# A tiled squared-ReLU attention ahead of two feed-forward layers: order of the products in an attention step, a tile's last step in two parts, another start

## The chip, the cores and the metric

The program runs on one core of a Trainium2 chip. The metric is the device time of one execution in microseconds (us), less is better. The engines are TensorE (PE; its weight loads are PEld), VectorE (DVE), ScalarE (ACT), GpSimd (POOL) and SyncE (SP), which issues nearly all the DMAs. Each works through its own instructions in order, and they wait for each other by semaphores.

## What is computed

```python
def _attn_ref(u, v, z):                     # u, v: (2, 3008, 256)   z: (2, 3008, 64)
    scores = (1.0 / 3008) * np.matmul(z, z.transpose(0, 2, 1))
    attn = np.maximum(scores, 0.0) ** 2
    return u * np.matmul(attn, v)

def _moe_ref(x, w_in, w_out):               # x: (6016, 256), 2048 hidden
    h = x @ w_in
    return (h - np.tanh(h)) @ w_out

def _moe2_ref(x, w_gate, w_val, w_out):     # 1536 hidden
    gate = 1.0 / (1.0 + np.exp(-(x @ w_gate)))
    return (gate * (x @ w_val)) @ w_out

def reference(...):
    return _moe2_ref(_moe_ref(_attn_ref(u, v, z).reshape(6016, 256), ...), ...)
```

## The kernel before

Every matmul operand is split in two: a high half (a rounded copy in fp32r) and a low half (what the rounding left). A product is three matmuls: high by high, high by low, low by high.

**Attention.** Twelve tiles `T` of 512 queries (448 in tiles 5 and 11), six per batch, each over 12 steps `p` of two chunks of 128 keys; `s = 12 T + p` counts 144 steps. `score(s)` (L428) computes z by z into two banks of `hidden`: a contraction of 64, so the matmuls come in pairs, one on the upper 64 rows of the array and one on the lower, three pairs a step. `attend(s)` (L453) multiplies the squared scores by v into `acc`: twelve pairs a step, three for each key chunk `c` and each half `d` of the output's 256 columns. The rows of a chunk are shared between the two array halves, so each `d` has two partial sums, `acc[d]` and `acc[2 + d]`. In a tile's last step 64 keys are padding and nine pairs do. PE's order is written by hand: `score(s + 2)`, then `attend(s)` (L584).

Between them ACT takes the relu of the scores (L712, "relu" below, into `first`, profile name `h`), waits until `attend(s - 2)` is done, and squares it into `part_hi` (L724, "square"). DVE squares in full precision (L902, into `full`, profile name `h`) and subtracts the high half from it, into `part_lo` (L915, by the helper at L799; "low half" below). `attend(s)` waits for the low half (`s_alo`, L476) before its first pair, since its second pair needs it.

**A tile's border.** When tile T is done, its partial sums are joined: ACT copies `acc[2 + d]` into `x_out` (L636), DVE adds `acc[d]` (L851, `s_sum`), d = 0 then 1. ACT does its copies in step 13 of the tile's count (`GATE_AT`: the next tile's p = 1) between relu and square, DVE its sums at the start of that step. The first half is signalled by PE (`s_half`) after five of the last step's nine pairs. PE may write the next tile's `acc[d]` only after `s_sum` (L479). One step later DVE multiplies by u (`gate_by_u`, L860), and SP stores the tile and loads the next u (L387).

**Beside it,** z and v are staged by DMA through three buffers and split into halves by "tasks" (ACT L624, DVE L799; table at L121): a task comes first in its step. The scores of tile 0 wait for the low half of z (L439). The weights of both layers are combined and split in the free time of DVE and ACT (`weight_steps`, L146; DVE L811 to L817 and L799) and stored by SP as `ready`; each unit's raw weights are loaded three steps ahead (L392).

**The start.** GpSimd clears `part_lo` (L613), and PE runs 8 warm-up pairs of 512 columns on it (L578), which compute nothing that is used, then `score(0)`, which waits for ACT's high half and later for DVE's low half of the first z piece.

**The two layers** follow (L589 on): products of x by weights into `hidden` (`product`, L424 to L426), activations on ACT and DVE, and second products into `acc`. The change leaves them alone.

## Time and profile before

| | us |
|---|---|
| three runs | 1509.5, 1510.15, 1510.15; median 1510.15 |
| the profiled execution | 1509.4 |
| its span, first to last instruction | 1507.6 |

| engine | busy, us | share of the span |
|---|---|---|
| PE | 1496.5 | 99% |
| PEld | 1312.2 | 87% |
| DVE | 1138.6 | 76% |
| ACT | 948.7 | 63% |

A pair of matmuls is recorded at some 0.39 us, but the next pair starts 0.23 us after it: matmuls are pipelined. So a gap in PE's work that is shorter than 0.16 us shows in no idle time, and a longer one shows shortened. It is seen from the starts of neighbouring rows, and from the idle time of PEld. The attention takes the first 486 us.

### The profile page before, as it was taken

Reading aid. Unit: us, or ns where it says so; the run is one execution under the profiler, and the core shown is the slowest. Engines: PE = TensorE matmul, PEld = TensorE weight load, DVE = VectorE, ACT = ScalarE, POOL = GpSimd, SP = SyncE. Lnnn points to the kernel's source line nnn. Section 1 sums busy time; section 2 is a strip of 40 time slices with the busy share of each in tenths; the row PEclk is TensorE's granted clock in tenths of the full one; section 3 lists DMA queues with packets and bytes.
Section 4 is the critical chain, followed back from the end, with each engine's and each line's share of the span. In section 5 each row is a group of like instructions: output and inputs, shape, how many; then the busy total and the mean of one; then the engine's idle time right before and its main releaser. Section 6 shows DMA issues by size and latency. Waiting matters only on the chain.

```text
span 1507.6 us, 21886 instructions
## 1 busy us (share of the span) xinstructions
PE 1496.5 (99%) x8800; PEld 1312.2 (87%) x8800; DVE 1138.6 (76%) x1409; ACT 948.7 (63%) x1282; POOL 0.7 (0%) x5
## 2 busy tenths in 40 slices
PE   9999999999999999999999999999999999999998
PEld 7999999999999788888888889888888888888897
DVE  8898888999987777767776767666666676666655
ACT  7676667767666666666666666656555555555654
POOL 0000000000000000000000000000000000000000
PEclk9999999999999999999999999999999999999999
DMA  4334432245333345354535446543635454554352
GB/s 133 130 124 154 154 120 88 104 168 219 126 120 142 122 149 209 125 200 154 188 137 191 157 158 233 201 174 140 241 129 208 162 195 175 189 184 183 135 207 87
DMA packets 36325, 241.79 MB, mean 160 GB/s; under 512 B 3584, under 2 KB 6656, under 8 KB 22912
## 3 DMA queue, kind: packets, MB, share of 16 engines
q1 hardware_dynamic: 36080, 240.17, 43.5%
q8 instruction: 69, 1.13, 0.3%
q14 instruction: 32, 0.26, 0.1%
q10 hardware_dynamic: 144, 0.23, 0.0%
HBM read 196.21 MB, written 44.17 MB: 159 GB/s over the span
## 4 chain that ended last, share of the span: by engine, by line
PE 98%; DVE 1%; ACT 0%; issue 0%; POOLq 0%; DVEq 0%
PE acc L470 25%; PE hidden L424 12%; PE hidden L426 12%; PE hidden L425 12%; PE acc L424 10%; PE acc L425 10%; PE acc L426 10%; PE hidden L447 6%; DVE part_lo L799 0%; PE acc L578 0%; DVE h L868 0%; DVE h L902 0%; ACT snap L665 0%; DVE region L799 0%; DVE h L894 0%
## 5 line engine op out<-in xcount | busy, mean ns | idle before, releaser
L799 DVE TENSOR_TENSOR part_lo<-h,part_hi 128x1024 fp32r<-128x1024 f32 (+2 forms) x315 | 375.4, 1192 | 91.8 <-ACT part_hi L676 49.4
L470 PE MATMUL acc<-part_hi,region 64*128 64x512 f32 (+1 forms) x2256 | 398.2, 384 | 2.0 <-DVE part_lo L799 1.6
L665 ACT ACTIVATE snap<-hidden 128x512 f32<-128x512 f32 (+1 forms) x360 | 211.7, 588 | 253.8 <-PE hidden L426 253.7
L424 PE MATMUL hidden<-region 128*128 128x512 f32 (+1 forms) x840 | 324.4, 386 | 2.6 <-ACT snap L665 1.9
L426 PE MATMUL hidden<-region 128*128 128x512 f32 (+1 forms) x840 | 323.7, 385 | 0.0
L425 PE MATMUL hidden<-region 128*128 128x512 f32 (+1 forms) x840 | 323.7, 385 | 0.0
L868 DVE TENSOR_TENSOR h<-hidden,snap 128x512 f32<-128x512 f32 (+1 forms) x252 | 170.9, 678 | 148.7 <-ACT snap L665 122.3
L470 PEld LDWEIGHTS acc<-part_hi,region 64*128 64x128 f32 x2256 | 258.5, 184 | 14.4 <-issue 7.0
L424 PE MATMUL acc<-part_hi,region 128*128 128x512 f32 (+1 forms) x672 | 259.2, 386 | 0.2 <-DVE part_lo L799 0.2
L425 PE MATMUL acc<-part_lo,region 128*128 128x512 f32 (+1 forms) x672 | 259.0, 385 | 0.0
L426 PE MATMUL acc<-part_hi,region 128*128 128x512 f32 (+1 forms) x672 | 258.9, 385 | 0.0
L470 PE MATMUL acc<-part_lo,region 64*128 64x512 f32 (+1 forms) x1128 | 250.5, 382 | 0.0
L724 ACT ACTIVATE part_hi<-h 128x1024 fp32r<-128x1024 f32 (+1 forms) x143 | 149.2, 1044 | 136.3 <-PE acc L470 136.1
L676 ACT ACTIVATE part_hi<-h 128x1024 fp32r<-128x1024 f32 (+1 forms) x166 | 172.9, 1042 | 81.5 <-DVE h L972 42.5
L424 PEld LDWEIGHTS hidden<-region 128*128 128x128 f32 x840 | 157.7, 188 | 35.0 <-ACT snap L665 3.7
L426 PEld LDWEIGHTS hidden<-region 128*128 128x128 f32 x840 | 157.7, 188 | 29.6
L425 PEld LDWEIGHTS hidden<-region 128*128 128x128 f32 x840 | 157.7, 188 | 29.4
L902 DVE TENSOR_TENSOR h<-h 128x1024 f32<-128x1024 f32 (+1 forms) x143 | 171.0, 1196 | 0.2 <-ACT h L712 0.2
L424 PEld LDWEIGHTS acc<-part_hi,region 128*128 128x128 f32 x672 | 126.1, 188 | 24.5 <-DVE part_lo L799 0.5
L426 PEld LDWEIGHTS acc<-part_hi,region 128*128 128x128 f32 x672 | 126.2, 188 | 23.8
L425 PEld LDWEIGHTS acc<-part_lo,region 128*128 128x128 f32 x672 | 126.2, 188 | 23.7
L712 ACT ACTIVATE h<-hidden 128x1024 f32<-128x1024 f32 (+1 forms) x143 | 141.6, 990 | 0.5 <-PE hidden L447 0.5
(56 smaller groups left out, 1185.7 us busy)
## 6 DMA issues: line engine op xcount, KB each, us to landing
region<-ready SPq DMA_DIRECT2D x33, 2304.0 KB, 8.8
region<-ready SPq DMA_DIRECT2D x51, 1408.0 KB, 6.0
ready<-region SPq DMA_DIRECT2D x6, 2304.0 KB, 7.4
ready<-region SPq DMA_DIRECT2D x8, 1408.0 KB, 5.6
xs<-x_out SPq DMA_DIRECT2D x20, 512.0 KB, 4.9
x_in<-xs SPq DMA_DIRECT2D x20, 512.0 KB, 7.9
snap<-vP SPq DMA_DIRECT2D x24, 256.0 KB, 2.7
u_in<-uT SPq DMA_DIRECT2D x10, 512.0 KB, 5.1
```

Of the source, the lines that this page charges most:

```text
L424: pe.matmul(dst, w_hi, x_hi, start=start, stop=False, skip_group_check=True)
L425: pe.matmul(dst, w_hi, x_lo, start=False, stop=False, skip_group_check=True)
L426: return pe.matmul(dst, w_lo, x_hi, start=False, stop=stop, skip_group_check=True)
L447: last = pe.matmul(hidden[:, 2 * (s % 2) + c, 0:w], keys_of[ROWS[c], keys], tokens_of[ROWS[c], tokens], start=i == 0, stop=i == 2, skip_gr ...
L470: last = pe.matmul(acc[:, 2 * r + d, 0:w], v[ROWS[r], 2 * p + c, half], a[ROWS[r], 2 * (s % 2) + c, 0:w], start=start, stop=False, skip_gr ...
L665: act.activation(snap[:, g % 2, i, 0:w], hidden[:, CHAIN[g % 2], 0:w], ACT.Copy).then_inc(s_snap, 1)
L676: act.activation(part_hi[:, b, 0:w], h[:, n % 2, b, 0:w], ACT.Copy).then_inc(s_hi, 1)
L712: act.activation(first[:, k, :, 0:w], hidden[:, 2 * k:2 * k + 2, 0:w], ACT.Relu, scale=1.0 / SEQ).then_inc(s_relu, 1)
L724: act.activation(part_hi[:, 2 * k:2 * k + 2, 0:w], first[:, k, :, 0:w], ACT.Square).then_inc(s_ahi, 1)
L799: return ve.tensor_tensor(dst, whole, hi.bitcast(F32), ALU.subtract)
L868: ve.tensor_tensor(dst, hidden[:, (BANK2, BANK7, BANK7)[i], 0:w], snap[:, g % 2, (0, 2, 1)[i], 0:w], ALU.add).then_inc(s_add, 1)
L902: ve.tensor_tensor(full[:, k, :, 0:w], first[:, k, :, 0:w], first[:, k, :, 0:w], ALU.mult).then_inc(s_full, 1)
```

## The change

The products of an attention step are put in another order: all that need the high half of the squared scores first (`highs`, two pairs each), then those that need the low half (`lows`, one pair). `highs` waits for `s_ahi` (ACT's square), `lows` for `s_alo`. Tile-first steps go by d, so that each d waits for its own `s_sum`.

A tile's last step is cut in two, after its fifth pair, where `s_half` is signalled, and `score(s + 2)` stands between the parts. ACT's copy of the first half moves ahead of the relu of the GATE_AT step; DVE's first sum moves one step earlier, between the full square and the low half of the next tile's first step; the second copy and sum stay in the GATE_AT step. `gate_by_u`, `store_tile` and `load_u` come one step later. The weights' and the second batch's tasks get other steps (`EARLY`, `late`, `X0_SPLIT`), none of them in the two steps around a border.

At the start the first z piece is split by DVE alone (a copy, then the subtraction, signalled by `s_zhi`), and the warm-up is 12 pairs of 256 columns on a half-size clear.

```diff
 NSTAGE = 3
-WARM = 8
+WARM = 12
...
+def steps_between(a, b):
+    return [s for s in range(a, b) if s not in GATE_AT and s + 1 not in GATE_AT]
+EARLY = steps_between(14, 60)
 def split_tasks():
...
     tasks += [(p, "v", (0, p)) for p in range(1, STEPS)]
-    tasks += [(at, "z", (1, k)) for k, at in enumerate((19, 31, 43, 55, 63, 65))]
-    later = [at for at in range(67, 81) if at not in GATE_AT and at - 1 not in GATE_AT]
-    tasks += [(at, "v", (1, p)) for p, at in enumerate(later)]
+    tasks += [(EARLY[5 * k + 4], "z", (1, k)) for k in range(ZP)]
+    tasks += [(at, "v", (1, p)) for p, at in enumerate(steps_between(67, 81))]
     return sorted(tasks, key=lambda t: t[0])
...
 def weight_steps():
-    free = [s for s in range(81, 125) if s not in GATE_AT and s - 1 not in GATE_AT]
+    late = steps_between(81, X0_LOAD)
     for k, pieces in enumerate(WPIECES):
         if WLAYER[k] == 0:
-            yield tuple(15 + 6 * k + i for i in range(2 + pieces))
+            yield tuple(EARLY[5 * k:5 * k + 4])
         else:
-            yield tuple(free.pop(0) for _ in range(2 + pieces))
+            yield tuple(late.pop(0) for _ in range(2 + pieces))
+X0_LOAD, X0_SUMS = 125, 127
+X0_SPLIT = (131, 134, 135, 136, 137, 138, 139)
 WSTEPS = tuple(weight_steps())
 WEIGHTS_AT = {s: (k, i) for k, steps in enumerate(WSTEPS) for i, s in enumerate(steps)}
-X0_LOAD, X0_SUMS = 125, 127
-X0_SPLIT = (131, 132, 135, 136, 137, 138, 139)
 assert max(WEIGHTS_AT) < X0_LOAD
...
                 for T in range(NT - 1):
-                    if s == GATE_AT[T] + 2:
+                    if s == GATE_AT[T] + 3:
                         store_tile(T)
...
                     piece = -(-2 * P * (p + 1) // ZW) - 1
-                    if p == 0 and T == 0:
-                        pe.wait_ge(s_thi, TASK_NUMBER["z", (b, piece)] + 1)
+                    if s == 0:
+                        pe.wait_ge(s_zhi, 1)
                     else:
...
-            def attend(s):
+            def pair(s, upper, lower, start=False):
...
                 w = tile_width(T)
...
+            def wait_v(s):
+                T, p = ORDER[s]
                 if T == 0 or T == TPB:
...
-                for c, d in whole:
-                    pe.wait_ge(s_alo, c + 1 if s == 0 else behind(s))
-                    if p == 0 and c == 0 and T > 0:
+            def highs(s, c, d):
+                T, p = ORDER[s]
+                pe.wait_ge(s_ahi, c + 1 if s == 0 else behind(s))
+                pair(s, (d, c, vh, part_hi), (d, c, vh, part_hi), p == 0 and c == 0)
+                return pair(s, (d, c, vl, part_hi), (d, c, vl, part_hi))
+            def lows(s, c, d):
+                pe.wait_ge(s_alo, c + 1 if s == 0 else behind(s))
+                return pair(s, (d, c, vh, part_lo), (d, c, vh, part_lo))
+            def attend(s):
+                T, p = ORDER[s]
+                wait_v(s)
+                if s == 0:
+                    for c in range(2):
+                        for d in range(DH):
+                            highs(s, c, d)
+                        for d in range(DH):
+                            last = lows(s, c, d)
+                elif p == 0:
+                    for d in range(DH):
                         pe.wait_ge(s_sum, 2 * (T - 1) + d + 1)
-                    if p == STEPS - 1 and c == 1:
-                        pair((0, c, vh, part_hi), (0, c, vh, part_lo))
-                        pair((0, c, vl, part_hi), (1, c, vl, part_hi)).then_inc(s_half, 1)
-                        continue
-                    for v, a in ((vh, part_hi), (vh, part_lo), (vl, part_hi)):
-                        last = pair((d, c, v, a), (d, c, v, a), p == 0 and c == 0 and v is vh
-                                    and a is part_hi)
-                if p == STEPS - 1:
-                    last = pair((1, 1, vh, part_hi), (1, 1, vh, part_lo))
+                        for c in range(2):
+                            highs(s, c, d)
+                        for c in range(2):
+                            last = lows(s, c, d)
+                else:
+                    for c in range(2):
+                        for d in range(DH):
+                            highs(s, c, d)
+                    for c in range(2):
+                        for d in range(DH):
+                            last = lows(s, c, d)
                 last.then_inc(s_attn, 1)
+            def attend_end_first(s):
+                wait_v(s)
+                highs(s, 0, 0)
+                lows(s, 0, 0)
+                pair(s, (0, 1, vh, part_hi), (0, 1, vh, part_lo))
+                pair(s, (0, 1, vl, part_hi), (1, 1, vl, part_hi)).then_inc(s_half, 1)
+            def attend_end_second(s):
+                highs(s, 0, 1)
+                lows(s, 0, 1)
+                pair(s, (1, 1, vh, part_hi), (1, 1, vh, part_lo)).then_inc(s_attn, 1)
             def product(n, s, i):
...
                 for r in range(2):
-                    pe.matmul(acc[:, 2 * r, :], part_lo[ROWS[r], 0, 0:P], part_lo[ROWS[r], 0, :],
-                              start=True, stop=True, skip_group_check=True)
+                    pe.matmul(acc[:, 2 * r, 0:256], part_lo[ROWS[r], 0, 0:P],
+                              part_lo[ROWS[r], 0, 0:256], start=True, stop=True,
+                              skip_group_check=True)
             score(0)
...
             for s in range(1, NSTEP - LAG):
-                score(s + LAG)
-                attend(s)
+                if ORDER[s][1] < STEPS - 1:
+                    score(s + LAG)
+                    attend(s)
+                else:
+                    attend_end_first(s)
+                    score(s + LAG)
+                    attend_end_second(s)
             attend(NSTEP - 2)
-            attend(NSTEP - 1)
+            attend_end_first(NSTEP - 1)
+            attend_end_second(NSTEP - 1)
             products_begin(0, 0)
...
-            gp.memset(part_lo[:, 0, :].bitcast(F32), 0.0).then_inc(s_zero, 1)
+            gp.memset(part_lo[:, 0, 0:256].bitcast(F32), 0.0).then_inc(s_zero, 1)
...
-            def copy_halves(T):
+            def copy_half(T, d):
...
                 for task in tasks_at(s):
-                    split_task(task)
+                    if task > 0:
+                        split_task(task)
+                if s in GATE_AT:
+                    copy_half(GATE_AT.index(s), 0)
                 if s == 0:
...
                 if s in GATE_AT:
-                    copy_halves(GATE_AT.index(s))
+                    copy_half(GATE_AT.index(s), 1)
                 act.wait_ge(s_relu, behind(s))
...
             def split_task(k):
                 whole, hi, lo = staged(k)
-                ve.wait_ge(s_thi, k + 1)
+                if k == 0:
+                    ve.wait_ge(s_stage[0], 16)
+                    ve.tensor_copy(hi, whole).then_inc(s_zhi, 1)
+                    ve.wait_ge(s_zhi, 1)
+                else:
+                    ve.wait_ge(s_thi, k)
                 minus(lo, whole, hi).then_inc(s_tlo, 1)
             def sum_weights(k, i):
...
-            def sum_halves(T):
+            def sum_half(T, d):
...
                 if s in GATE_AT:
-                    sum_halves(GATE_AT.index(s))
+                    sum_half(GATE_AT.index(s), 1)
                 if s == 0:
...
                     split_x(0, X0_SPLIT.index(s))
+                if s + 1 in GATE_AT:
+                    sum_half(GATE_AT.index(s + 1), 0)
                 ve.wait_ge(s_full, behind(s))
...
                       part_hi[:, 2 * k:2 * k + 2, 0:w]).then_inc(s_alo, 1)
-                if s - 1 in GATE_AT:
-                    gate_by_u(GATE_AT.index(s - 1))
+                if s - 2 in GATE_AT:
+                    gate_by_u(GATE_AT.index(s - 2))
```

In PE's order at the first border, from the score of step 13 (before) or from the last whole step of tile 0 (after), to the next tile's first step; `hidden` rows are scores, `acc` rows are `attend`. Before:

```order
L447 MATMUL hidden<-region 128x512 x6
L470 MATMUL acc<-part_hi,region 128x512 x2
L470 MATMUL acc<-part_lo,region 128x512 x2
L470 MATMUL acc<-part_hi,region 128x512 x3
L470 MATMUL acc<-part_lo,region 128x512
L470 MATMUL acc<-part_hi,region 128x512 x4
L470 MATMUL acc<-part_lo,region 128x512 x2
L470 MATMUL acc<-part_hi,region 128x512 x3
L470 MATMUL acc<-part_lo,region 128x512
L447 MATMUL hidden<-region 128x512 x6
L470 MATMUL acc<-part_hi,region 128x512 x2
```

After:

```order
L468 MATMUL acc<-part_hi,region 128x512 x4
L468 MATMUL acc<-part_lo,region 128x512 x2
L468 MATMUL acc<-part_hi,region 128x512
L468 MATMUL acc<-part_lo,region 128x512
L468 MATMUL acc<-part_hi,region 128x512 x2
L455 MATMUL hidden<-region 128x512 x6
L468 MATMUL acc<-part_hi,region 128x512 x4
L468 MATMUL acc<-part_lo,region 128x512 x2
L468 MATMUL acc<-part_hi,region 128x512
L468 MATMUL acc<-part_lo,region 128x512
L455 MATMUL hidden<-region 128x512 x6
L468 MATMUL acc<-part_hi,region 128x512 x8
```

The score of step 13 has moved from before the last step into its middle.

In DVE's order at the same border (the `x_out` rows are the sums and, at 128x2x512, the product by u; `h` is the full square, `raw` are weights). Before:

```order
L902 TENSOR_TENSOR h<-h 128x1024
L799 TENSOR_TENSOR part_lo<-h,part_hi 128x1024
L851 TENSOR_TENSOR x_out<-acc,x_out 128x512 x2
L902 TENSOR_TENSOR h<-h 128x1024
L799 TENSOR_TENSOR part_lo<-h,part_hi 128x1024
L902 TENSOR_TENSOR h<-h 128x1024
L799 TENSOR_TENSOR part_lo<-h,part_hi 128x1024
L860 TENSOR_TENSOR x_out<-x_out,u_in 128x2x512
```

After:

```order
L955 TENSOR_TENSOR h<-h 128x1024
L904 TENSOR_TENSOR x_out<-acc,x_out 128x512
L847 TENSOR_TENSOR part_lo<-h,part_hi 128x1024
L904 TENSOR_TENSOR x_out<-acc,x_out 128x512
L955 TENSOR_TENSOR h<-h 128x1024
L847 TENSOR_TENSOR part_lo<-h,part_hi 128x1024
L955 TENSOR_TENSOR h<-h 128x1024
L865 TENSOR_TENSOR raw<-raw 128x128
L866 TENSOR_TENSOR raw<-raw 128x128
L847 TENSOR_TENSOR part_lo<-h,part_hi 128x1024
```

The first sum now stands ahead of the low half of step 12, the second behind it.

DVE's first instructions, before and then after:

```order
L799 TENSOR_TENSOR region<-snap,region 128x512 x3
L894 TENSOR_TENSOR h<-h 128x512
L799 TENSOR_TENSOR part_lo<-h,part_hi 128x512
L894 TENSOR_TENSOR h<-h 128x512
L799 TENSOR_TENSOR part_lo<-h,part_hi 128x512
```

```order
L854 CAST region<-snap 128x512
L847 TENSOR_TENSOR region<-snap,region 128x512 x3
L947 TENSOR_TENSOR h<-h 128x512
L847 TENSOR_TENSOR part_lo<-h,part_hi 128x512
L947 TENSOR_TENSOR h<-h 128x512
```

One instruction is added ahead of the three subtractions.

## Rows read from the trace of the kernel before

**Rows 1.** The page: engines' totals; then one of PE's waits: us, times, longest.
```profile
PE 1496.5 (99%) x8800; PEld 1312.2 (87%) x8800; DVE 1138.6 (76%) x1409; ACT 948.7 (63%) x1282; POOL 0.7 (0%) x5
...
PE acc L470 <- DVE part_lo L799: 1.6, 1, 1.6
```

**Rows 2.** Idle time before attend's PE instructions, in us, and the number of times.
```profile
  issue: 7.0, 13
```

**Rows 3.** Timeline, first border: start us, duration us, engine, instruction [idle before].
```profile
47.59 0.88 PE L447 MATMUL hidden<-region 64*128 64x512 f32 x6
47.89 1.06 ACT L724 ACTIVATE part_hi<-h 128x1024 fp32r<-128x1024 f32 x1 [1.43 <-PE acc L470]
...
48.85 1.01 ACT L712 ACTIVATE h<-hidden 128x1024 f32<-128x1024 f32 x1
...
49.76 0.59 ACT L636 ACTIVATE x_out<-acc 128x512 f32<-128x512 f32 x1
...
50.31 0.88 PE L447 MATMUL hidden<-region 64*128 64x512 f32 x6
50.38 1.49 DVE L851 TENSOR_TENSOR x_out<-acc,x_out 128x512 f32<-128x512 f32 x2
...
51.22 0.50 PE L470 MATMUL acc<-part_hi,region 64*128 64x512 f32 x2
51.52 0.43 PE L470 MATMUL acc<-part_lo,region 64*128 64x512 f32 x2
```

**Rows 4.** Timeline of PEld where it restarts behind tiles 1 and 5.
```profile
91.63 0.21 PEld L470 LDWEIGHTS acc<-part_hi,region 64*128 64x128 f32 x2 [0.42 <-issue]
...
249.90 0.22 PEld L470 LDWEIGHTS acc<-part_hi,region 64*128 64x128 f32 x2 [0.50 <-issue]
```

**Rows 5.** Timeline of PE, two undisturbed steps apart.
```profile
54.04 0.87 PE L447 MATMUL hidden<-region 64*128 64x512 f32 x6
...
55.17 0.64 PE L470 MATMUL acc<-part_hi,region 64*128 64x512 f32 x4
55.63 0.42 PE L470 MATMUL acc<-part_lo,region 64*128 64x512 f32 x2
...
57.44 0.87 PE L447 MATMUL hidden<-region 64*128 64x512 f32 x6
```

**Rows 6.** Groups by line and shape, attention: count | busy us, mean ns.
```profile
L799 DVE TENSOR_TENSOR part_lo<-h,part_hi 128x1024 fp32r<-128x1024 f32 x119 | 145.8, 1225 | 32.4 <-ACT part_hi L724 30.3
...
L851 DVE TENSOR_TENSOR x_out<-acc,x_out 128x512 f32<-128x512 f32 x20 | 13.8, 692 | 2.5 <-ACT x_out L636 0.8
```

**Rows 7.** The chain that ended last, up to 16.4 us: start us, us, what.
```profile
1.31 3.78 PE acc L578 x12
...
6.19 0.60 ACT h L703
...
6.81 0.70 DVE h L894
...
15.67 0.61 DVE region L799
```

**Rows 8.** Timeline of the start.
```profile
3.55 1.28 ACT L624 ACTIVATE region<-snap 128x512 fp32r<-128x512 f32 x2 [1.53 <-DMA snap<-zT]
...
4.89 1.94 PE L447 MATMUL hidden<-region 64*128 64x512 f32 x12
...
5.87 0.69 DVE L799 TENSOR_TENSOR region<-snap,region 128x512 fp32r<-128x512 f32 x1 [0.31 <-ACT region L624]
```

**Rows 9.** Timeline of PEld at the start of the attention's last step.
```profile
484.41 0.19 PEld L470 LDWEIGHTS acc<-part_hi,region 64*128 64x128 f32 x2 [0.24 <-DVE part_lo L799]
...
484.72 0.39 PEld L470 LDWEIGHTS acc<-part_hi,region 64*128 64x128 f32 x3
```

**Rows 10.** SP's timeline: a load of raw weights behind a border.
```profile
379.21 0.86 SPq L316 DMA_DIRECT2D x_in<-w  x1
```

**Rows 11.** The page's DMA issues: count, KB each, median us to landing.
```profile
x_in<-w SPq DMA_DIRECT2D x3, 1280.0 KB, 8.3
```

55 lines of the change are left out of this document (25 added, 30 removed).

## The prediction

> **What bounds the kernel now.** Start with the totals: PE is busy for 1496.5 of 1507.6 us, DVE for 76% [rows 1]. So no edit that leaves PE's products alone can bring more than the few us in which PE stands still or runs slowly. The list of waits names almost nothing for the attention (1.6 us behind DVE at the start [rows 1]), but it hides short gaps, since a pair of matmuls is drawn at 0.39 us and the next starts earlier. So the pitch comes next: from one score to the next score an undisturbed step takes 57.44 - 54.04 = 3.40 us for 15 pairs, 0.2267 us a pair [rows 5]. Against that pitch the timeline of a tile's border is read [rows 3]. The score of step 14 starts at 50.31; three pairs later, at 50.99, `attend(12)` could start. It starts at 51.22, 0.23 late, and its second pair follows after 0.30 instead of 0.23 (an emptied PE needs 0.07 to refill). That is 0.30 us lost. What ended last: DVE's first sum, 50.38 plus 0.69 [rows 6] = 51.07, and 0.15 until PE moves. PE's weight loads restart from 0.42 us idle at the next border too, and from 0.50 behind tile 5 [rows 4]; attend's instructions have 13 such gaps with 7.0 us idle in all [rows 2], eleven at the eleven borders and two at the start. Lost at the borders: 10 x 0.30 + 0.38 = 3.4 us.
>
> The start is a second place. PE runs warm-up until the first score at 4.89 [rows 8], and from 6.81 to 16.29 the chain of waits runs through DVE alone: sums of squares, low halves, splits of z and v, with no PE in it [rows 7]. Then PE gets the next z piece at 16.4. Third: `attend(143)`, the last step, waits for its low half: PEld idles 0.24 us at 484.41, and the pair behind comes 0.31 later instead of 0.20, some 0.17 us lost in all [rows 9].
>
> **The change part by part.** *The border.* I lay the new order on the old times, from 47.59, where attend(10) ends [rows 3]. PE: five pairs of attend(11), of which the fifth (it signals `s_half`) starts at 48.50 and has drained at 48.92; three pairs of score, to 49.41; four pairs of attend(11), to 50.31; three of score, to 50.99; then attend(12). No pair is added. ACT: the square of step 12 runs 47.89 to 48.95 as before [rows 3], so the copy, now ahead of the relu, runs 48.96 to 49.55. DVE's first sum (0.69) ends at 50.27; with 0.15 to PE it is there at 50.42, and 50.99 is when it is wanted: 0.57 to spare, where 0.23 was missing. Then DVE must do the low half of step 12 (1.23 [rows 6]): 50.24 to 51.47, with 0.15 at PE at 51.62. In the old order of products that would have stopped PE again, since its second pair needs it at 51.22. In the new one, four pairs of high halves go first and it is wanted at 51.90: the two parts of the change need each other. ACT's second copy comes behind the relu (scores drained 49.60, relu to 50.65, copy to 51.2), DVE's second sum behind the low half: 51.4 to 52.1, at PE 52.25. The second d starts six pairs into the step, at 52.35. With the 0.07 of refill that is a tie: the cost lies between 0 and 0.07 us a border. I take 0.02, because each time above is rounded against the change. Border: 3.4 - 11 x 0.02 = **3.2 us** won; ends 2.6 and 3.4.
>
> *The moves around it.* ACT's copy now stands ahead of a relu that PE's later scores wait for; that relu comes 0.8 later than at 48.85 and is wanted only by score(15), at 53.7. Behind DVE's new wait (some 1.5 us idle for the copy) are queued the low half of step 12, the second sum and the full square of step 13. DVE leaves the border about 1.3 us behind its old times. It is wanted by PE for low halves, which are now needed eight pairs (1.8 us) into a step, and it has 3.40 us for 2.45 us of squares and low halves plus 0.6 to 0.9 of splitting; `gate_by_u` (1.2 us) moves one step back, still before the backlog reaches 1.8 + 1.4 us of slack. So 0. `store_tile`, `load_u` and, queued behind them on SP, the raw weights of the units that load there come about 3.4 us later. The tightest of them is the unit of 1280 KB whose load issues at 379.21 [rows 10]: it comes to stand directly behind the product by u and two DMA issues (1.3 us), a load of its size and place lands 8.3 us after its issue [rows 11], and its first use is three steps and a full square (10.2 + 1.2) after that product. So 9.6 us of 11.4 are used: the cover is 1.8 us, and if it is gone, DVE stands still, and PE only once the low half is 1.8 us later still. Cost 0, price if wrong: about 1 us for each of five such loads.
>
> *The order inside a step.* Same pairs, same weights, other banks: PE changes the `acc` bank after one or two pairs instead of three. Unknown as such; the nearest rows are four matmuls that cross a bank, 55.17 to 55.63, 0.46 for two pairs [rows 5], which is the 0.23 of any pair. Taken 0; bounds -0.2 and +0.5 us over all.
>
> *The start.* The copy that DVE adds is not in the trace. Its bounds are nothing and a subtraction of the same tile, 0.69 [rows 8]; I take the upper end. DVE starts when ACT did, at 3.55: high half 4.25, PE's first score pair at 4.4; low half 4.95, second pair 5.1, third 5.5 at the half-speed pitch of 0.43 that the warm-up shows (the relu now starts 1.29 after the first pair, two such pitches and one drain), relu at 5.95 instead of 6.19 [rows 7]. DVE is then busy with the third split until 6.56 [rows 8], so its first square starts at 6.57 instead of 6.81. From there on the chain is DVE's and 0.24 is carried through to 16.4; one relu that it met at its own end comes earlier too, for 0.1 more. That PE runs attend(0) and attend(1) about 1 us earlier (high halves come before low halves) brings nothing, because the next score waits for DVE's split of z. Start: **0.3 us** won; ends 0 and 0.9.
> The Trainium skill (VectorE: DVE Perf Modes, "The perf-mode tier table") has a 32-bit copy in SBUF at twice the rate of a `tensor_tensor`; by it the copy would be an estimated 0.4 us, the relu would start 0.1 earlier, ACT's third split would then hold it, and the start would be worth 0.3 still. No row here shows that copy.
>
> *The attention's last step.* The low half is wanted two pairs later, by more than it was late: **0.17 us** won.
>
> Sum: 3.2 + 0.3 + 0.2 = 3.7 us. 1509.4 of the profiled execution, 1.8 of it outside the span, becomes 1505.7. The four times of the kernel before have a mean of 1509.8, 0.35 under the median; I forecast **1506.1** for the median after. In the two layers nothing is changed, and PE's few gaps there are behind its own products, so they move with it.
>
> **The rivals.** *The second sum replaces the first.* If the tie above goes against the change by 0.1 to 0.2 us (a copy that waits longer behind the relu, a wait that costs DVE 0.1), each border keeps 0.15 us: gain 3.7 - 1.5 = 2.2, 1507.6. For it: the slack of 0.03. Against it: only that sum is so tight, and eleven borders are alike.
> *The clock.* Eight warm-up pairs take 3.78 us [rows 7], 0.43 each: 512 columns at 1.2 GHz. The six pairs of the first two scores take 1.94 [rows 8], which is two pitches of 0.43, three of 0.23 and a drain, so PE works at 2.4 GHz from about 5.7 us, after 4.4 us without a gap. The new warm-up ends near 3.9 us and leaves PE idle for 0.5 before the first score. If the rise comes later for that, each pair at the lower level costs 0.2 more, but up to 16 us PE has over 1 us in hand. A rise at 9 us costs under 0.2, one at 12.5 about 0.4: 1506.3 to 1506.5.
> The Trainium skill (TensorE: Matmul & The Clock Gate, "The HAM clock gate") says that the moment of the rise varies between runs; the one trace here can't show that.
> *The change does not do what it says:* PE's gap is at the border for another reason than the first sum, such as the order of banks or the square. Then the borders stay as they are: 1509.3. Against it: 51.07 and 51.22 are 0.15 apart, the distance of every start of PE behind DVE.
> *Slower.* PE pays for changing the `acc` bank. There are some four more changes a step, in 144 steps 570; from 6 ns each the gain of 3.7 is gone, and at 12 ns the time is 1509.8 + 3.1 = 1513. For it: no stretch of this kernel changes banks with every pair as the low halves now do. Against it: two pairs across a change take 0.46 [rows 5].
> *More.* The start goes by PE and not by DVE: 0.9 instead of 0.3, 1505.5; a small chance.
>
> **How the numbers follow.** About 0.2%, 3.0 us, is what a measurement of this kernel can tell from no change. Forecast (1505.3 to 1507.0): 0.57, all but 0.04 of it faster by over 0.2%. Second sum: 0.20, two thirds of it within 0.2%. Late clock: 0.06, half of it within. More: 0.06, faster. Not what it says, or a late DMA that eats the gain: 0.06, within. Slower: 0.05. Sum: faster 0.69, same 0.26, slower 0.05; one third of the cases are short of the forecast and few beyond it, so the range is lopsided: 1505.0 to 1508.7, which leaves out half of "more", the case without gain and the slower one.
>
> **What would show it.** In the profile after: PEld's idle time before attend's instructions at the borders gone (7.0 us down to under 3); the distance from tile to tile down from 91.63 - 51.19 (weights loaded 0.03 ahead of the 51.22 of [rows 3]) = 40.44 to 177 pairs x 0.2267 = 40.13 us; the first sum ended some 0.6 us before attend(12) starts; no gap six pairs into that step; PE's start behind the first z wait at 16.1 instead of 16.4; no gap at the attention's last step; the pitch of a step still 3.40. The forecast is wrong if the pitch is above 3.41, if a gap stands at each border's fourth or sixth pair, or if DVE's waits for raw weights show up.

## The result, and the profile after

| | before | after |
|---|---|---|
| median, us (20 runs each) | 1509.62 | 1507.05 |
| lowest and highest | 1508.47, 1510.15 | 1506.24, 1509.03 |
| the profiled execution, and its span | 1509.4, 1507.6 | 1506.3, 1504.5 |
| first product of the layers starts | 486.43 | 484.24 |

The ratio is 0.9985, 95% interval 0.9979 to 0.9991: 2.6 us faster, 0.17%. That is a gain that can be measured, but less than the 3.7 us forecast, and just under the 0.2% that the prediction counted as faster. The time lies 1 us above the number forecast and inside the range.

**The borders.** The first border again, now of the kernel after (start us, duration us, engine, instruction [idle before]):

```profile
47.51 1.06 ACT L771 ACTIVATE part_hi<-h 128x1024 fp32r<-128x1024 f32 x1 [1.43 <-PE acc L468]
...
48.36 0.87 PE L455 MATMUL hidden<-region 64*128 64x512 f32 x6
48.59 0.60 ACT L680 ACTIVATE x_out<-acc 128x512 f32<-128x512 f32 x1
...
49.22 0.69 DVE L904 TENSOR_TENSOR x_out<-acc,x_out 128x512 f32<-128x512 f32 x1 [1.58 <-ACT x_out L680]
...
49.82 1.22 DVE L847 TENSOR_TENSOR part_lo<-h,part_hi 128x1024 fp32r<-128x1024 f32 x1
49.95 0.87 PE L455 MATMUL hidden<-region 64*128 64x512 f32 x6
...
50.63 1.10 PE L468 MATMUL acc<-part_hi,region 64*128 64x512 f32 x8
...
50.96 0.69 DVE L904 TENSOR_TENSOR x_out<-acc,x_out 128x512 f32<-128x512 f32 x1
...
51.53 0.64 PE L468 MATMUL acc<-part_lo,region 64*128 64x512 f32 x4
...
51.99 0.87 PE L468 MATMUL acc<-part_hi,region 64*128 64x512 f32 x6
```

Against [rows 3]: the score starts at 49.95 and `attend(12)` at 50.63, three pairs of 0.227 later, with no gap. The first sum ended at 49.91, 0.72 early, where in [rows 3] PE had to wait 0.23 for it. The second sum ends at 51.65, and the second d starts at 51.99, six pairs after 50.63: it was a tie on paper and is none in the trace. The low half ends at 51.04 and is wanted at 51.53. So the four pairs of high halves, the two of low halves and the second d follow each other at an even pitch, and the changes of the `acc` bank cost nothing.

What attend's weight loads waited for, over the whole kernel after (us, times):

```profile
  DVE part_lo L847: 2.0, 1
  DVE region L847: 1.0, 1
```

The 7.0 us in 13 places of [rows 2] are gone. One new entry of 2.0 us stands there, and it is the surprise of this case.

**The new gap.** Timeline of SP, DVE and PE of the kernel after, at steps 124 to 128; then the same place of the kernel before:

```profile
418.06 0.55 SPq L372 DMA_DIRECT2D xs<-x_out  x1
418.65 0.62 SPq L376 DMA_DIRECT2D u_in<-uT  x1
419.86 0.33 SPq L330 DMA_DIRECT2D ready<-region  x1
420.31 2.11 SPq L367 DMA_DIRECT2D x_in<-xs  x2
...
433.08 0.69 DVE L885 TENSOR_TENSOR x_in<-x_in 128x512 f32<-128x512 f32 x1 [5.35 <-DMA x_in<-xs]
...
434.97 1.20 PE L468 MATMUL acc<-part_lo,region 64*128 64x512 f32 x8 [1.56 <-DVE part_lo L847]
```

```profile
418.39 0.55 SPq L364 DMA_DIRECT2D xs<-x_out  x1
418.99 0.62 SPq L368 DMA_DIRECT2D u_in<-uT  x1
423.14 0.33 SPq L322 DMA_DIRECT2D ready<-region  x1
423.59 1.31 SPq L359 DMA_DIRECT2D x_in<-xs  x2
...
433.56 0.69 DVE L831 TENSOR_TENSOR x_in<-x_in 128x512 f32<-128x512 f32 x1 [1.60 <-DMA x_in<-xs]
```

`load_x(0)` fetches the first batch's rows for the layers; DVE adds them up from step `X0_SUMS` = 127 on. Before, its first transfer was issued 4.6 us behind the u load, and the second landed 9.55 us after its own issue. After, `store_tile` and `load_u` stand one step later, directly ahead of it: it is issued 1.7 us behind the u load, with the tile's store (landed 421.41), the u load (423.80), a `ready` store and its own two halves all under way at once, and the second lands 12.27 us after its issue (420.79 to 433.06). Before, the u load had landed at 423.50, ahead of the first transfer's issue. DVE sits idle for 5.35 us in front of the first row sum. The low half of step 127 is queued behind that sum, ends at 434.9, and PE has stood still since its last high half: the starts of neighbouring pairs are 2.02 apart at 432.95, then 0.34. That is 1.9 us lost once per execution.

**The start.** Timeline of the kernel after:

```profile
3.53 0.43 DVE L854 CAST region<-snap 128x512 fp32r<-128x512 f32 x1 [3.53 <-DMA snap<-zT]
...
4.01 2.77 PE L455 MATMUL hidden<-region 64*128 64x512 f32 x12
...
16.13 0.96 PE L455 MATMUL hidden<-region 64*128 64x512 f32 x6 [1.62 <-DVE region L847]
```

The z wait ends at 16.13 instead of 16.42, the 0.3 us of the forecast. DVE's copy took 0.43 us.

**From the two traces to the medians.** To the start of the layers: 486.43 - 484.24 = 2.2 us. Read from the starts of all pairs, the borders gave 3.7, the start 0.3, the last step 0.2, and the new gap took 1.9: 2.3. The layers themselves, from their first product to the last (1502.82 before, 1499.70 after), took 0.93 us less in this execution. Nothing of the change lies there, and in ten of the eleven other traces below the layers took 1016.2 to 1016.4, like the 1016.4 before: the mean distance of some 750 neighbouring 448-column matmuls was 204.3 ns in the one and 203.3 in the other, 0.7 us in all. So these two executions are 3.1 us apart and the medians 2.6.

### The profile page after: what moved, and what is told of

Read it like the earlier page. It is cut to its first block, busy times and chain, and to the rows that moved or that the text cites. A ratio compares the mean times of both kernels' runs of the same rounds, so it can differ in the third digit from the quotient of the medians.

```text
span 1504.5 us, 21902 instructions
## 1 busy us (share of the span) xinstructions
PE 1492.4 (99%) x8808; PEld 1304.1 (87%) x8808; DVE 1134.1 (75%) x1410; ACT 948.6 (63%) x1281; POOL 0.5 (0%) x5
## 4 chain that ended last, share of the span: by engine, by line
PE 96%; DVE 2%; DMA 1%; ACT 0%; issue 0%; SPq 0%; DVEq 0%
PE acc L468 23%; PE hidden L432 12%; PE hidden L433 12%; PE hidden L434 12%; PE acc L432 10%; PE acc L433 10%; PE acc L434 10%; PE hidden L455 6%; DMA x_in<-xs 1%; DVE part_lo L847 1%; DVE h L955 0%; DVE region L847 0%; DMA snap<-zT 0%; DVE h L921 0%; ACT snap L709 0%
## 5 line engine op out<-in xcount | busy, mean ns | idle before, releaser
L468 PE MATMUL acc<-part_hi,region 64*128 64x512 f32 (+1 forms) x2256 | 291.5, 382 | 0.6 <-ACT part_hi L753 0.6
L468 PEld LDWEIGHTS acc<-part_hi,region 64*128 64x128 f32 x2256 | 242.9, 184 | 13.3 <-DVE region L847 1.0
L468 PE MATMUL acc<-part_lo,region 64*128 64x512 f32 (+1 forms) x1128 | 161.6, 383 | 1.6 <-DVE part_lo L847 1.6
```

What stands on the lines that cost most here:

```text
L468: last = pe.matmul(acc[:, 2 * r + d, 0:w], v[ROWS[r], 2 * p + c, half], a[ROWS[r], 2 * (s % 2) + c, 0:w], start=start, stop=False, skip_gr ...
```

## The experiments

All against the kernel before, whose median beside them was 1509.6 to 1509.7. First the new gap, then the two parts of the border, then the start.

**The first batch's sums two steps later.** The changed kernel with

```diff
-X0_LOAD, X0_SUMS = 125, 127
-X0_SPLIT = (131, 134, 135, 136, 137, 138, 139)
+X0_LOAD, X0_SUMS = 125, 129
+X0_SPLIT = (134, 135, 136, 137, 138, 139, 140)
```

> The changed kernel with the four sums of x0 two steps later (steps 129 to 132) and its seven splits at steps 134 to 140; the load stays at step 125. Both theories: the load has landed (433.1) when DVE gets to step 129 (about 434), so DVE waits for it under 0.5 us, PE has no gap at 433, the layers start near 482.3 us and the time is 1.9 us under the changed kernel's, some 4.4 us under the kernel before. If instead a sum in step 132, beside the tile's first sum, upsets the border, a gap of up to 0.7 us stands at 455 to 458.

Measured: 1504.53 us (1504.45 to 1505.29), ratio 0.9967, interval 0.9954 to 0.9979. The load is as late as before, 12.26 us from issue to landing, but DVE asks for it later; its row sum has no idle time before it, and the step around it runs on:

```profile
432.13 1.22 DVE L847 TENSOR_TENSOR part_lo<-h,part_hi 128x1024 fp32r<-128x1024 f32 x1 [1.04 <-ACT part_hi L771]
433.20 1.08 PE L468 MATMUL acc<-part_lo,region 64*128 64x512 f32 x8
...
434.41 0.68 DVE L885 TENSOR_TENSOR x_in<-x_in 128x512 f32<-128x512 f32 x1
```

The gap came from the late load, and with it gone the gain is 5.1 us.

**The same two kernels side by side.** The changed kernel as it is, and the one with the later sums, once more on one chip:

> The changed kernel unchanged, beside the same with the later first-batch sums, on one chip. Theory (one gap of 1.9 us at the load of the first batch's rows): 1507.0, the gap stands again near 433 with the load landing 12 us after its issue, and 2.0 to 2.7 us above the kernel with the later sums. Rival (the low time of that kernel was a favourable chip or run): the two differ by less than 1 us.

> The changed kernel with its first-batch sums two steps later (129 instead of 127) and the splits behind them, once more. Theory: 1504.5, no gap near 433; the 448-column pairs at 203 to 206 ns as in every execution so far, which over some 353 attention pairs and 752 of the last layer block moves a single execution by up to 1 us either way. Rival: it comes out within 1 us of the changed kernel.

Measured: 1506.88 (1506.03 to 1507.51), ratio 0.9981, interval 0.9972 to 0.9990, against 1504.90 (1503.85 to 1505.03), ratio 0.9968, interval 0.9956 to 0.9980. The two differ by 2.0 us; all 6 runs of the one are faster than all 11 of the other. The gap stood again in the first (1.88 us at 433.88, load landed 12.29 after issue) and in the second not. So some 1.9 us is a steady price of the changed kernel.

**Product by u, store and next u back one step early.** The changed kernel with

```diff
-                    if s == GATE_AT[T] + 3:
+                    if s == GATE_AT[T] + 2:
                         store_tile(T)
...
-                if s - 2 in GATE_AT:
-                    gate_by_u(GATE_AT.index(s - 2))
+                if s - 1 in GATE_AT:
+                    gate_by_u(GATE_AT.index(s - 1))
```

> The changed kernel with one part undone: gate_by_u, store_tile and load_u stand one step earlier again, as in the kernel before. Its trace showed a new gap of 1.9 us (PE at 432.95 to 434.97) where DVE waits 5.35 us for the load of x0, against 1.6 us before. Theory A: the tile's store and the load of u, issued 1.2 us ahead of the last weights' store, make the x load land 12.3 us after its issue instead of 9.5. Then here the latency is near 9.5, DVE waits under 2.5 us, PE's gap at about 433 is gone, the first product of the layers starts near 482.3 us instead of 484.2, and the time is 1.9 us under the changed kernel's. Rival B: PE is simply 3.7 us earlier and a DMA that takes as long as ever comes late for it; then the latency doesn't matter, DVE still waits over 4 us and PE's gap stays at 1 us or more.

Measured: 1510.71 us, ratio 1.0008, interval 0.9999 to 1.0017. The load at step 125 landed 9.57 after its issue again, DVE waited 2.57 for it, and the gap at 433 was gone: theory A, and not B. But the time missed the expectation by over 5 us, since the same collision came up elsewhere, at step 111, and cost more. Timeline of this kernel:

```profile
374.88 0.54 SPq L372 DMA_DIRECT2D xs<-x_out  x1
375.47 0.61 SPq L376 DMA_DIRECT2D u_in<-uT  x1
376.13 0.85 SPq L330 DMA_DIRECT2D ready<-region  x1
377.02 0.51 SPq L324 DMA_DIRECT2D x_in<-w  x1
...
386.44 0.68 ACT L689 ACTIVATE region<-raw 128x576 fp32r<-128x576 f32 x1 [7.30 <-DMA ready<-region]
...
388.12 2.93 PE L468 MATMUL acc<-part_hi,region 64*128 64x512 f32 x16 [3.57 <-ACT part_hi L771]
```

A `ready` store of weights now stood directly behind the tile's store and the u load, since the change's `late` steps had moved its unit's last piece from step 108 to 110. It took 10.2 us, and ACT waited 7.3 us to write into the buffer that it frees. The square is queued behind that, so this time PE stopped for the high half, 3.8 us. Then came a second bill. The stretches around it (us, busy time and count of PE, PEld, DVE, ACT, POOL, granted clock, DMA share, GB/s):

```profile
384.00:389.00 5.00, 1.43 (x14) 0.86 (x12) 1.59 (x2) 2.56 (x4) 0.00 (x0) 1.00 0.84 356
389.00:393.00 4.00, 4.00 (x24) 3.17 (x22) 4.00 (x5) 3.13 (x5) 0.00 (x0) 0.57 0.02 4
393.00:397.00 4.00, 4.00 (x38) 3.60 (x38) 4.00 (x5) 3.10 (x4) 0.00 (x0) 1.00 0.00 0
```

PE started again at 388.12 and ran for 1 us at its usual pitch; then its granted clock was 0.57 on average over four microseconds: eight pairs came at 0.427 us instead of 0.227, which is 1.2 GHz instead of 2.4, and cost another 1.6 us. The Trainium skill (TensorE: Matmul & The Clock Gate, "The HAM clock gate") says that the clock is lowered again after idle time. Here 3.8 us of it did so; behind the 1.9 us of the gap at 433 the pairs stayed 0.227 apart.

So moving the store by a step is neither good nor bad as such; each place has its own transfers behind it. In the traces the layers start 6.1 us later here than with the later sums, and 5.4 of that are this stop with the slow pairs behind it. (The layers then took 1.25 us less in this one execution, by the distance of their 448-column matmuls; the medians are 6.2 apart.)

**The border part alone, sum ahead of the low half.** The kernel before, with its order of products, the last step in two parts around the score, the first copy ahead of the relu, and the sum ahead of the low half:

```diff
-                attend(s)
+                if ORDER[s][1] < STEPS - 1:
+                    score(s + LAG)
+                    attend(s)
+                else:
+                    attend(s, 0)
+                    score(s + LAG)
+                    attend(s, 1)
...
+                if s + 1 in GATE_AT:
+                    sum_half(GATE_AT.index(s + 1), 0)
                 ve.wait_ge(s_full, behind(s))
                 ve.wait_ge(s_ahi, behind(s))
                 minus(part_lo[:, 2 * k:2 * k + 2, 0:w], full[:, k, :, 0:w],
                       part_hi[:, 2 * k:2 * k + 2, 0:w]).then_inc(s_alo, 1)
```

> The kernel before with the border's part alone: last step in two parts around the score, first copy ahead of relu, first sum ahead of the low half of the next tile's first step. The products inside a step keep their old order (low half wanted by the second pair), and start, weights and gate_by_u stay as before. Theory: the two parts of the change need each other. The low half of step 12, behind the sum, reaches PE at about 51.5, 0.5 to 0.6 us after attend(12) could start, so each border shows a gap of 0.6 to 0.7 us instead of 0.30 and the time is 3 to 4.5 us ABOVE the kernel before. Rival: the gap at the border was the sum alone; then the gaps go and the time is some 3.3 us below.

Measured: 1512.2 us, ratio 1.0014, interval 1.0005 to 1.0023. The second border of this kernel:

```profile
91.11 1.21 DVE L809 TENSOR_TENSOR part_lo<-h,part_hi 128x1024 fp32r<-128x1024 f32 x1
...
92.38 0.51 PE L470 MATMUL acc<-part_hi,region 64*128 64x512 f32 x2 [0.28 <-DVE part_lo L809]
```

PE is ready at 91.94 and starts at 92.38, behind the low half that ended at 92.32. Each border loses 0.44 plus 0.11 of refill instead of 0.30: the low half is late in the place of the sum. That is 2.5 us in all, less than the 3 to 4.5 expected: PE starts 0.055 us behind the low half at ten of the eleven borders, where 0.15 had been put in.

**The border part alone, sum behind the low half.** The same kernel with

```diff
-                if s + 1 in GATE_AT:
-                    sum_half(GATE_AT.index(s + 1), 0)
                 ve.wait_ge(s_full, behind(s))
...
                       part_hi[:, 2 * k:2 * k + 2, 0:w]).then_inc(s_alo, 1)
+                if s + 1 in GATE_AT:
+                    sum_half(GATE_AT.index(s + 1), 0)
```

> As the border's part alone, but DVE does the first sum behind the low half of the next tile's first step instead of ahead of it. Theory: low half at 50.3 as before, sum 50.3 to 50.9, at PE 51.05 with 0.07 of refill against a start at 50.99: a gap of 0.1 to 0.15 us at each border instead of 0.30, so 1.7 to 2.2 us below the kernel before. Rival (every wait at the border costs the same 0.3, since PE empties anyway): gaps of 0.3, no change.

Measured: 1507.02 us (1505.83 to 1507.58), ratio 0.9983, interval 0.9974 to 0.9991. The second border here:

```profile
88.81 0.60 ACT L643 ACTIVATE x_out<-acc 128x512 f32<-128x512 f32 x1
88.90 1.23 DVE L809 TENSOR_TENSOR part_lo<-h,part_hi 128x1024 fp32r<-128x1024 f32 x1 [0.24 <-ACT part_hi L733]
...
90.04 0.68 DVE L860 TENSOR_TENSOR x_out<-acc,x_out 128x512 f32<-128x512 f32 x1
90.19 0.84 PE L447 MATMUL hidden<-region 64*128 64x512 f32 x6
...
90.87 0.50 PE L470 MATMUL acc<-part_hi,region 64*128 64x512 f32 x2
```

DVE fills the time in which it would wait for the copy with the low half. The sum ends at 90.72, PE wants it at 90.87. The gaps are gone but for 0.08 us between attend's first two pairs. From the starts of all pairs, ten borders keep 0.1 to 0.17 us each and tile 5's 0.46, 1.6 us in all of the 3.7 before. The time is 2.6 us below the kernel before, more than the 1.7 to 2.2 expected; 0.4 of that is the z wait of this trace. The whole change brought no more, but only because it lost 1.9 us at its late load.

**Later sums of the rows, and the border sum behind the low half.** The new order of products, with the same move of these two lines, on top of the kernel with the later row sums:

> The kernel with the later first-batch sums, and DVE's first border sum moved from ahead of the low half of the next tile's first step to behind it. Theory (the place of the sum does not matter once ACT copies ahead of the relu): ACT's copy still ends near 49.2, DVE does the low half 48.6 to 49.8, then the first sum to about 50.5, and PE wants it at 50.63. So no gap at the borders, or one of up to 0.1 us, and the low half is done 1.2 us earlier than before. Time 1504.5 to 1505.6. Rival (the order inside DVE decides, as in the kernel with the old order of products): the sum comes 0.2 us or more late at each of eleven borders, 2 to 4 us in all, 1506.7 or more.

Measured: 1504.94 us (1504.75 to 1505.02), ratio 0.9969, interval 0.9958 to 0.9981, and 1504.90 for its neighbour with the sum ahead. Timeline of the first border:

```profile
48.69 1.23 DVE L847 TENSOR_TENSOR part_lo<-h,part_hi 128x1024 fp32r<-128x1024 f32 x1 [1.03 <-ACT part_hi L771]
...
49.83 0.68 DVE L904 TENSOR_TENSOR x_out<-acc,x_out 128x512 f32<-128x512 f32 x1
...
50.63 1.14 PE L468 MATMUL acc<-part_hi,region 64*128 64x512 f32 x8
```

The sum ends at 50.51 and PE starts on time at 50.63. With the high halves first, both orders of DVE do; with the old order of products only one does. So the new order of products buys freedom for DVE at a border. It buys time as well: with DVE's work in this same order, the eleven borders keep 0.2 us here (all of it at tile 5's) and 1.6 with the old order of products, and the time is 1504.94 against 1507.02, of which the row load at 433 explains no more than 0.1.

**The order of products alone.** The kernel before with `highs` and `lows` as in the change, the last step in one piece behind its score, nothing else:

```diff
                 score(s + LAG)
-                attend(s)
+                if ORDER[s][1] < STEPS - 1:
+                    attend(s)
+                else:
+                    attend_end_first(s)
+                    attend_end_second(s)
```

> The kernel before with the new order of products inside a step alone (high halves first; the last step in the new order too but not parted by a score). Theory: the gaps at the eleven borders (0.30 us each) stay, since the first d still waits for its sum; the gap of 0.17 us at 484.4 goes; up to 16.4 us nothing is gained, since DVE sets the first z wait. Pitch of a step 3.40 us as before. Time 0.2 us below the kernel before: no difference that can be measured. Rival (changing the acc bank with nearly every pair costs): pitch above 3.41 and a time over 2 us above.

Measured: 1507.90 us (1506.41 to 1508.32), ratio 0.9988, interval 0.9979 to 0.9996: 1.8 us, not the 0.2 expected. Part of it shows at the borders, which should not have changed. The second border of this kernel, then of the kernel before:

```profile
90.34 1.49 DVE L886 TENSOR_TENSOR x_out<-acc,x_out 128x512 f32<-128x512 f32 x2
...
91.09 1.20 PE L460 MATMUL acc<-part_hi,region 64*128 64x512 f32 x8
```

```profile
90.82 1.49 DVE L851 TENSOR_TENSOR x_out<-acc,x_out 128x512 f32<-128x512 f32 x2
...
91.66 0.50 PE L470 MATMUL acc<-part_hi,region 64*128 64x512 f32 x2
```

By the raw records the first sum ends at 91.03 here and at 91.51 there, and PE starts 0.06 and 0.15 behind it. The gap at a border, with its refill, is 0.21 instead of 0.30, 0.9 us over ten borders. Tile 5's border lost 0.29 instead of 0.54, the last step lost 0.2 less, and the z wait ended 0.34 earlier (which, as shown below, is the execution and not the kernel). So 1.3 to 1.4 of the 1.8 us are found and the rest is not. Why PE follows the sum 0.09 sooner when four pairs of high halves stand behind that wait instead of one, no run separates.

**The start alone.** The kernel before with 12 warm-up pairs of 256 columns and DVE's copy of the first z piece:

```diff
-WARM = 8
+WARM = 12
...
+                if k == 0:
+                    ve.wait_ge(s_stage[0], 16)
+                    ve.tensor_copy(hi, whole).then_inc(s_zhi, 1)
```

> The kernel before with the start's part alone (DVE splits the first z piece, 12 warm-up pairs of 256 columns). Theory: attend(0) starts some 0.2 us earlier (it still waits for the low half), DVE's chain 0.2 to 0.3 us earlier, PE's first z wait ends 0.2 to 0.3 us earlier than 16.42, everything else as before; time 0.3 us below, not measurable. Rival (the clock's rise comes later in some runs): runs with a mean clock of 0.998 or less that are 2 us longer than the others.

Measured: 1509.49 us, ratio 0.9998, interval 0.9989 to 1.0007; the z wait ended at 16.15. The 0.27 us in the trace are below what so many runs can tell from nothing.

**The old warm-up under the new start.** The kernel with the later sums, with 8 warm-up pairs of 512 columns as before:

```diff
-WARM = 12
+WARM = 8
...
-                    pe.matmul(acc[:, 2 * r, 0:256], part_lo[ROWS[r], 0, 0:P],
-                              part_lo[ROWS[r], 0, 0:256], start=True, stop=True,
-                              skip_group_check=True)
+                    pe.matmul(acc[:, 2 * r, :], part_lo[ROWS[r], 0, 0:P], part_lo[ROWS[r], 0, :],
+                              start=True, stop=True, skip_group_check=True)
```

> The changed kernel with the sums of x0 two steps later (1504.5 us) and the old warm-up (8 pairs of 512 columns on a full-size clear). The first z piece is still split by DVE. Theory: PE is in the warm-up until 4.9 us, so the first score starts at 4.9 instead of 4.0, its relu near 6.2 instead of 6.0, and PE's first z wait ends 0.2 us later than with the short warm-up: +0.2 us, not measurable. Rival: the short warm-up costs a later rise of the clock, and the old one is as fast or faster.

Measured: 1505.91 us (1505.51 to 1506.48), ratio 0.9975, interval 0.9966 to 0.9985, and the z wait ended at 16.54. A second thing showed that has nothing to do with the start:

```profile
310.62 0.69 ACT L688 ACTIVATE region<-x_in 128x576 fp32r<-128x576 f32 x1 [3.84 <-DMA ready<-region]
...
312.31 0.99 PEld L468 LDWEIGHTS acc<-part_hi,region 64*128 64x128 f32 x10 [0.54 <-ACT part_hi L770]
```

This is the wait of step 111 again, at another `ready` store (step 89) behind a tile's store and u load. In this execution the u load's issue took 1.44 us on SP instead of 0.62, the `ready` store was issued 2.08 us behind the tile's store instead of 1.81, and took 9.8 us instead of 9.5. PE lost 0.58. In the kernel with the later sums nothing stopped there, and its repeat lost 0.2. So after the change this place has no cover left, and 0.1 to 0.3 us on SP or in the DMA engines decide. This profiled execution and that of the kernel with the later sums are 2.0 us apart; most of the rest is 0.38 at the z wait and 448-column pairs 205.4 ns apart instead of 202.7 in the attention, 0.9 us. The medians are 1.4 apart, where 0.2 was expected, and all ten runs lie above all eleven of the two takes of the later sums, so a difference of the kernels there is. Which of the three terms it is can't be told from one trace each; the rival (the old warm-up is as fast) is out.

**GpSimd splits v in tile 0.** The start is bound by DVE, and GpSimd is idle. The kernel with the later sums, with the low halves of v's first-batch pieces 1 to 11 on GpSimd and the z pieces one step earlier:

```diff
+            for k in POOLED:
+                whole, hi, lo = staged(k)
+                gp.wait_ge(s_thi, k)
+                gp.tensor_tensor(lo, whole, hi.bitcast(F32), ALU.subtract).then_inc(s_plo, 1)
```

> The changed kernel with the sums of x0 two steps later, and in tile 0 the low halves of v (p = 1 to 11) computed by GpSimd instead of DVE, and the tasks of z one step earlier. Aimed at the last gap of the attention: PE waits 1.9 us at 14.0 to 16.1 for DVE's split of z. Theory (tile 0 is bound by DVE alone): the gap falls to under 0.3 us and the small ones at 23, 30 and 37 go: 1.5 to 2.1 us below 1504.5. Rival (GpSimd slows DVE or is too slow for v): the subtraction takes over 3 us on GpSimd, or DVE's squares take over 1.3 us beside it, and the gap stays or moves to the wait for v.

Measured: 1507.74 us, ratio 0.9987, interval 0.9979 to 0.9996, so 3.2 us slower than without. Groups of the first 45 us (count | busy us, mean ns):

```profile
L668 POOL TENSOR_TENSOR region<-snap,region 128x512 fp32r<-128x512 f32 x11 | 20.4, 1859 | 23.1 <-ACT region L679 23.1
L857 DVE TENSOR_TENSOR part_lo<-h,part_hi 128x1024 fp32r<-128x1024 f32 x9 | 16.9, 1878 | 0.3
...
L966 DVE TENSOR_TENSOR h<-h 128x1024 f32<-128x1024 f32 x10 | 13.8, 1376 | 0.5 <-ACT h L769 0.5
```

The z wait, 1.9 us of standstill before, shrank to 0.41. But a subtraction that DVE does in 0.69 takes GpSimd 1.86, and beside it DVE's own work stretches: the low half takes 1.88 on average against 1.23 [rows 6]. The Trainium skill (SBUF — State Buffer, "SBUF: two separate sides") says that GpSimd and a DVE operation with two SBUF inputs exclude each other from one pair of ports for a whole instruction, whoever starts first. The trace agrees one by one. A DVE square begun at 14.32 took its usual 1.21; GpSimd's subtraction, begun at 14.39, ended 1.16 after that square, at 16.69. DVE's low half, begun at 15.57 while GpSimd was at it, ended 1.09 behind GpSimd, 2.21 long, and five more low halves begun in the same place took 2.20 to 2.21. All eleven GpSimd subtractions began during a DVE instruction and ended 1.15 to 1.19 behind it. So GpSimd's own part is an estimated 1.16 us, and the rest of its 1.86 is waiting for DVE. PE then lost 0.4 to 1.0 us at five other places of tile 0.

## Why the prediction came out as it did

**The bound and the borders: right.** The gaps were where the timeline and the weight loads' idle times put them, and they were due to the first sum. 3.2 us was forecast for them and 3.7 measured: all that was lost came back, refills included, and it was more than the 3.4 put down (tile 5's border lost 0.54 and not 0.38, the ten others 0.30 to 0.35). The tie at the second sum, counted as 0.02 a border, went fully to the change. The pitch of a step stayed at 3.40, the distance of two tiles fell to 40.12 (forecast 40.13), and the rivals of the second sum, of the banks and of "not what it says" are out.

**"The two parts of the change need each other": half right.** With DVE's sum ahead of the low half they do: without the new order of products the border part made the kernel slower, 1512.2. With the sum behind the low half they don't: it brought 2.6 us by itself, the order of products 1.8 by itself, and with the start (0.2) that is about the 4.7 to 5.1 of all together with the late load out of the way. The prediction laid out one order of DVE's work and took its result for the border's. Its 0.15 us as "the distance of every start of PE behind DVE" doesn't hold either: it is 0.146 at all eleven borders of the kernel before, but 0.055 at ten borders of the kernel with the sum ahead.

**The start: the right size in the two traces, a third of it on average.** The copy took 0.43 us and not the 0.69 put in as upper end; the estimate by the Trainium skill (VectorE: DVE Perf Modes, "The perf-mode tier table") was 0.4, and the trace agrees. The sum was the same by both, since the chain hangs on DVE's later splits. But [rows 7] and [rows 8] are one execution, and two things differ from one to the next: when the first z piece is there to be split (3.34 to 3.75 us), and when PE comes to full speed. All executions with tile 0's plan unchanged, from the timelines:

| kernel | split of the first z piece starts | z wait ended | from the one to the other |
|---|---|---|---|
| before | 3.55 | 16.42 | 12.87 |
| border part, sum ahead | 3.57 | 16.64 | 13.07 |
| border part, sum behind | 3.42 | 16.03 | 12.61 |
| order of products alone | 3.49 | 16.09 | 12.60 |
| start alone | 3.44 | 16.15 | 12.71 |
| after | 3.53 | 16.13 | 12.60 |
| after, repeat | 3.75 | 16.51 | 12.76 |
| later sums | 3.34 | 16.16 | 12.82 |
| later sums, repeat | 3.42 | 16.02 | 12.60 |
| later sums, sum behind | 3.43 | 16.12 | 12.69 |
| product by u early | 3.45 | 16.05 | 12.60 |
| later sums, old warm-up | 3.44 | 16.54 | 13.10 |

The four with the old start have a mean of 12.79, the seven with the new one 12.68: 0.1 us of the forecast's 0.3 is left. The lowest value, 12.60, is reached by both. Before, where the row of the first two scores is 1.94 long [rows 8], PE ran at half speed until 5.7; with the sum ahead that row is 2.30 long, with the sum behind 1.54. So an old start is as good as a new one when the clock rises early, and up to 0.5 worse when it rises late. What the new start brings is less dependence on that moment. But the moment isn't all: with the later sums PE's pairs were 0.23 apart from 5.4 on, the earliest of the new starts, and 12.82 is their longest. What made it so is not known. With the old warm-up under the new copy the first two scores took 2.74, half speed until 7.0, and that gave the worst start of all.
The Trainium skill (TensorE: Matmul & The Clock Gate, "The HAM clock gate") says that the moment of the rise varies between runs of one kernel; these traces agree.

**The late clock: seen, at the price forecast.** It is the repeat of the changed kernel:

```profile
4.24 3.23 PE L455 MATMUL hidden<-region 64*128 64x512 f32 x12 [0.21 <-DVE region L854]
7.62 2.02 PE L468 MATMUL acc<-part_hi,region 64*128 64x512 f32 x8 [0.16 <-ACT part_hi L753]
9.46 0.65 PE L468 MATMUL acc<-part_lo,region 64*128 64x512 f32 x4
```

PE idled for 0.4 us ahead of the first score, and its pairs stayed 0.43 apart until 9.4 us; in the kernel after they were 0.23 apart from 6.2 on. The z wait ended 0.38 later than there, of which 0.22 is the z piece's later landing. That leaves 0.16, where the prediction had "a rise at 9 us costs under 0.2".

**The order of banks and the last step: right.** Nothing and 0.2 us.

**The step that failed: "the moves around it … So 0".** It followed what `store_tile` and `load_u` push back on SP, but only to the raw weights. There nothing was lost: the load of [rows 10] landed 9.6 us after its issue in the kernel after, not 8.3, but DVE first used it 5.5 us after that (388.81, 394.33), where the prediction had a cover of 1.8, and no wait of DVE for raw weights shows. `load_x(0)` at step 125 was not looked at. It stands one step behind the new place of the last store, is two transfers of 512 KB, and DVE waited 1.6 us for it already in the kernel before. The prediction's closing list had the symptom (DVE's waits) for raw weights only. The price per late load was put at about 1 us; it was 1.9. "A late DMA that eats the gain" had a share of a chance of 0.06. A second place, the `ready` store of step 89, also lost its cover, but costs only 0 to 0.6 us.

By terms: 3.7 forecast, 0.5 more at the borders, 0.2 less at the start, 1.9 lost at the load: 2.1, where 2.6 was measured, with an interval from 1.4 to 3.2. The time lies in the range because the range was wide enough on the slow side, which the second sum had been given; it is not that rival that came true.

**What stays open.** The single times of the changed kernel spread from 1506.2 to 1509.0. A late z piece, a late rise of the clock, the `ready` store of step 89 and the pitch of the 448-column pairs each move one execution by 0.2 to 1 us, as the traces show; which of them made the highest times can't be said, since the traces are of other executions. That PE starts 0.09 us sooner behind a sum in the new order of products, and as soon behind a low half in the old one, is not explained either.

## What to carry to other kernels

When a step moves, list every transfer issued within two steps behind its new place, whoever it belongs to, with what its consumer waited for in the old trace: the one that already shows a wait is the first to break. A wait at the head of an in-order engine can be repaired by asking later: here that gave back all of it, while moving the transfers in front of the late one broke another place. And when work must come ahead of other work, lay out both orders on the engine that does it: the one that fills the wait for its input gave most of the gain here without the second change.

## What the runs showed of the hardware

- A pause of 3.8 us brought PE's granted clock down, 1 us after PE had started again, to 0.57 on average over four microseconds (eight pairs at 0.427 us); pauses of 1.8 to 1.9 us did not.
- Transfers issued close together delayed each other by over a quarter: the second of two row loads of 512 KB landed 9.6 us after its issue when the next tile's u had been asked for 5.0 us ahead (two traces), and 12.1 to 12.3 us when 2.1 us ahead (four traces). SP's own issue of it took 1.4 to 1.6 us instead of 0.9.
- A DVE fp32 copy of 128x512 in SBUF takes 0.43 us, a `tensor_tensor` of that size 0.69.
- GpSimd and DVE beside each other took turns by whole instructions: DVE's low half took 2.20 to 2.21 us instead of 1.23 when begun during GpSimd's subtraction (1.88 on average), and each of the eleven subtractions ended 1.15 to 1.19 us after the DVE instruction begun before it.
- A PE whose pipeline has run dry takes 0.08 to 0.11 us more for its next pair.
- Pairs of 448 columns are not equally far apart in each execution: their mean in the attention was 202.7 to 205.4 ns (512 columns: 226.7 to 226.9). Over some 350 pairs of the attention this moves an execution by up to 1 us, and so do the some 750 matmuls of that width in the layers (202.7 to 204.3 ns), whatever the kernel. A single profiled execution cannot be held against another to better than that.
